# Routing, row sums, key transposes and sink values issued in another order on VectorE, and one more attention tile computed in halves

## The reference

```python
# q, k, v: (4, 8, 768, 64); n_sink = 4; window = 128
scores = scale * np.matmul(q, k.transpose(0, 1, 3, 2))
keep = is_sink | in_window            # in_window: 0 <= rel < window
a = softmax(np.where(keep, scores, -1e9))
x = np.matmul(a, v)                   # as (3072, 512)

a = x @ w1; b = x @ w2                # 512 x 1024 each
x = ((a * b) @ w3) @ w_out            # 1024 x 1024, 1024 x 512

logits = x @ w_gate + modality_bias[modality_id]
e_idx = np.argmax(logits, axis=1)     # one expert of 8 for each token
out[mask] = gate_w[mask, None] * (np.maximum(x[mask] @ w1[e], 0.0) @ w2[e])
```

## Time and profile before

| | us |
|---|---|
| median of three runs | 913.49 |
| lowest and highest run | 912.72, 914.9 |
| the profiled execution's own time | 913.49 |
| its span in the profile | 911.9 |
| TensorE busy | 891.8 |
| VectorE busy | 613.7 |
| ScalarE busy | 383.9 |
| GpSimd busy | 176.9 |

### The profile page before, as it was taken

The page is one execution under the profiler, slowest core; times in us unless marked ns, Lnnn a source line. Parts: engine busy times, 40 slices in busy tenths (PEclk is TensorE's granted clock), DMA queues, the critical chain, the costliest instruction groups (busy, mean ns, idle before and its releaser), DMA issues.

```text
span 911.9 us, 22277 instructions
## 1 busy us (share of the span) xinstructions
PE 891.8 (98%) x8114; PEld 832.1 (91%) x8114; DVE 613.7 (67%) x1469; ACT 383.9 (42%) x933; POOL 176.9 (19%) x289
## 2 busy tenths in 40 slices
PE   7999999999999999999999999999999999999995
PEld 6778999999999999999999999999999999999994
DVE  6776776785776785785786763287666666666655
ACT  3556433342342443333333332251555555444553
POOL 2451112222221241221231221011100000000000
PEclk9999999999999999999999999999999999999998
DMA  7634623123123222222222212234711116111110
GB/s 225 203 116 163 213 66 102 37 92 96 48 87 87 70 71 71 71 83 68 82 71 70 71 48 70 82 140 140 255 46 46 46 58 218 47 47 44 40 40 27
DMA packets 80184, 83.39 MB, mean 91 GB/s; under 512 B 46303, under 2 KB 56543, under 8 KB 80096
## 3 DMA queue, kind: packets, MB, share of 16 engines
q1 hardware_dynamic: 75568, 68.54, 24.4%
q0 software_dynamic: 4240, 13.66, 4.0%
q10 hardware_dynamic: 288, 0.00, 0.0%
HBM read 56.70 MB, written 25.74 MB: 90 GB/s over the span
## 4 chain that ended last, share of the span: by engine, by line
PE 93%; DVE 2%; issue 1%; ACT 1%; DMA 1%; DVEq 0%; ACTq 0%; POOL 0%; SPq 0%; POOLq 0%
PE acc_a L335 7%; PE acc_b L335 6%; PE acc_b L336 6%; PE acc_b L337 6%; PE acc_a L337 6%; PE acc_a L336 6%; PE misc L329 4%; PE misc L331 4%; PE misc L330 4%; PE s_even L949 3%; PE acc_a L329 3%; PE attn L330 2%; PE acc_b L329 2%; PE attn L331 2%; PE attn L329 2%; PE acc_a L331 2%
## 5 line engine op out<-in xcount | busy, mean ns | idle before, releaser
L816 POOL TENSOR_TENSOR probs<-scores,row_inv 128x256 f32<-128x256 f32 x96 | 66.4, 711 | 287.1 <-DVE row_inv L1881 287.1
L1373 ACT ACTIVATE ew<-raw_e 128x1024 fp32r (+1 forms) x100 | 101.3, 1050 | 13.8 <-issue 13.8
L335 PE MATMUL acc_a<-xT_w,w 128*128 128x384 f32 x256 | 90.2, 352 | 0.0
L335 PE MATMUL acc_b<-xT_w,w 128*128 128x384 f32 x256 | 88.0, 344 | 0.4 <-DVE ab L1933 0.4
L336 PE MATMUL acc_a<-xT_w,w 128*128 128x384 f32 x256 | 86.5, 338 | 0.0
L337 PE MATMUL acc_a<-xT_w,w 128*128 128x384 f32 x256 | 86.5, 338 | 0.0
L336 PE MATMUL acc_b<-xT_w,w 128*128 128x384 f32 x256 | 86.5, 338 | 0.0
L337 PE MATMUL acc_b<-xT_w,w 128*128 128x384 f32 x256 | 86.4, 338 | 0.0
L1399 ACT ACTIVATE scores<-scores,neg_max 128x136 f32<-128x136 f32 x192 | 75.8, 398 | 11.3 <-DVE neg_max L1871 11.1
L1373 ACT ACTIVATE uT_w<-ab 128x384 fp32r<-128x384 f32 x64 | 33.4, 521 | 110.5 <-DVE ab L1933 110.5
L2023 DVE TENSOR_TENSOR ew<-raw_e,ew 128x1024 fp32r<-128x1024 f32 x52 | 60.4, 1220 | 28.8 <-ACT ew L1373 28.8
(11 more groups left out here) (371 smaller groups left out, 2966.0 us busy)
## 6 DMA issues: line engine op xcount, KB each, us to landing
raw_e<-in_moe_w SPq DMA_DIRECT2D x24, 512.0 KB, 6.5
raw<-in_moe_w SPq DMA_DIRECT2D x16, 512.0 KB, 6.3
x_in<-routed SPq DMA_DIRECT2D x29, 257.0 KB, 2.9
v_nat<-in_v SPq DMA_DIRECT2D x24, 256.0 KB, 3.0
x_mid<-x_out SPq DMA_DIRECT2D x24, 256.0 KB, 2.0
x_in<-x_mid SPq DMA_DIRECT2D x24, 256.0 KB, 2.7
q_nat<-in_q SPq DMA_DIRECT2D x80, 64.0 KB, 2.2
k_nat<-in_k SPq DMA_DIRECT2D x80, 64.0 KB, 1.9
```

Of the source, the lines that this page charges most:

```text
L335: pe.matmul(o, w_hi, x_hi, start=start, stop=False, skip_group_check=True)
L816: pool.tensor_tensor(probs[:, at, side * HALF:(side + 1) * HALF], scores[:, at, side, SINKS:], row_inv[:, at].unsqueeze(2).broadcast_to([P ...
L1373: return act.activation(o, i, ACT.Copy)
```

## The change

Five things are moved or added. On DVE, `route_place(g - 1)` goes from behind `mlp_uT(g, 0)` to behind `mask_scores(ta, 1)`, and `sums(ta, 0)` goes ahead of `mlp_u(g, 0)`. `take_v_sinks`, which runs in turns 1, 3 and 5, goes from ahead of `mlp_u(g, 3)` to behind `mlp_uT(g, 4)`. `turn_qk` transposes k ahead of q, for 20 tiles; what needs k alone waits for two transposes now, and `scale_q` for all four. Tile 22 is halved, and PE then waits for `first_known` ahead of writing `misc` there.

```diff
--- before.py
+++ after.py
@@ -311,7 +311,7 @@
                 self.par, self.half = i % 2, self.no // 2
                 self.third = self.no // GT
                 self.by_pe = self.no < BY_PE
-                self.halved = self.no >= BY_PE and i >= 1 and self.no != TILES - 2
+                self.halved = self.no >= BY_PE and i >= 1
                 self.second = (s_odd, misc, s_odd)[self.no % GT]
                 self.turns = 4 * (self.no - BY_PE)
                 self.banks_used = self.no + min(self.no, BY_PE)
@@ -801,7 +801,7 @@
                 if t.by_pe:
                     pool.wait_ge(right_empty, 2 * t.no + 1)
                 else:
-                    pool.wait_ge(qk_turned, t.turns + 4)
+                    pool.wait_ge(qk_turned, t.turns + 2)
                 if t.no >= 1:
                     pool.wait_ge(scores_full, 4 * t.no)
                 own = keys[:, t.par, :, 2:5:2, SINKS:]
@@ -932,7 +932,7 @@
                     pe.wait_ge(left_empty, 2 * t.no + 1)
                     pe.wait_ge(right_empty, 2 * t.no + 1)
                 else:
-                    pe.wait_ge(qk_turned, t.turns + 4)
+                    pe.wait_ge(qk_turned, t.turns + 2)
                     pe.wait_ge(left_empty, t.banks_used)
                     pe.wait_ge(right_empty, t.banks_used)
                 pe.wait_ge(k_sink_ready, t.b + 1)
@@ -983,6 +983,8 @@
                     if t.second is misc:
                         pe.wait_ge(wg_taken, FOLD)
                         pe.wait_ge(rank_read, t.third - 1)
+                        if t.third == GROUPS - 1:
+                            pe.wait_ge(first_known, 1)
                     before, own = ((i - 1) % 3, before_probsT), (i % 3, own_probsT)
                     for c in range(PAIRS):
                         for half, (slot, pT), q0, q1 in ((0, own, 0, P), (1, before, 0, P), (0, before, 0, HALF), (1, own, HALF, P)):
@@ -1386,7 +1388,7 @@
                     .then_inc(right_empty, 1)
 
             def scale_q(t):
-                act.wait_ge(qk_turned, t.turns + 2)
+                act.wait_ge(qk_turned, t.turns + 4)
                 act.activation(qT[:, :, :], qT[:, :, :], ACT.Copy, scale=SCALE).then_inc(q_ready, 1)
 
             def exps(t, g):
@@ -1821,18 +1823,18 @@
                 ve.wait_ge(qk_in, 32 * BY_PE + 32 * t.turns + 128)
                 ve.wait_ge(scores_full, 4 * t.no)
                 for a in range(2):
+                    ve.transpose(keys[:, t.par, 2 * a:2 * a + 2, 2:5:2, SINKS:].rearrange("p e m (j f) -> p e f m j", f=4),
+                                 k_nat[:, a * 256:(a + 1) * 256].rearrange("p (f n e) -> p e f n", f=4, e=2)).then_inc(qk_turned, 1)
+                for a in range(2):
                     ve.transpose(qT[:, 2 * a:2 * a + 2, :].rearrange("p e (j f) -> p e f j", f=4),
                                  q_nat[:, a * 256:(a + 1) * 256].rearrange("p (f n e) -> p e f n", f=4, e=2)).then_inc(qk_turned, 1)
-                for a in range(2):
-                    ve.transpose(keys[:, t.par, 2 * a:2 * a + 2, 2:5:2, SINKS:].rearrange("p e m (j f) -> p e f m j", f=4),
-                                 k_nat[:, a * 256:(a + 1) * 256].rearrange("p (f n e) -> p e f n", f=4, e=2)).then_inc(qk_turned, 1)
 
             def take_k_sinks(t, b):
 
                 if t.by_pe:
                     ve.wait_ge(right_empty, 2 * t.no + 1)
                 else:
-                    ve.wait_ge(qk_turned, t.turns + 4)
+                    ve.wait_ge(qk_turned, t.turns + 2)
                 src = keys[:, 0, :, 2:3, SINKS:2 * SINKS].broadcast_to([P, PAIRS, 5, SINKS])
                 ve.tensor_copy(keys[:, 0, :, :, 0:SINKS], src)
                 ve.tensor_copy(keys[:, 1, :, :, 0:SINKS], src).then_inc(k_sink_ready, 1)
@@ -2123,14 +2125,14 @@
                 ta, tb, tc = (group_tile(g + 1, j) for j in range(GT))
                 mask_scores(ta, 0)
                 mask_scores(ta, 1)
+                if g > 0:
+                    route_place(g - 1)
+                sums(ta, 0)
                 mlp_u(g, 0)
                 if g == 0:
                     gate_weights(FOLD - 2)
-                sums(ta, 0)
                 sums(ta, 1)
                 mlp_uT(g, 0)
-                if g > 0:
-                    route_place(g - 1)
                 mlp_u(g, 1)
                 mlp_uT(g, 1)
                 take_probsT(ta, 0)
@@ -2141,8 +2143,6 @@
                 if g == 0:
                     gate_weights(FOLD - 1)
                 sum_x(ta)
-                if tb.i == 1:
-                    take_v_sinks(tb.b)
                 mlp_u(g, 3)
                 mlp_uT(g, 3)
                 mask_scores(tb, 0)
@@ -2151,6 +2151,8 @@
                 mlp_u(g, 4)
                 sums(tb, 1)
                 mlp_uT(g, 4)
+                if tb.i == 1:
+                    take_v_sinks(tb.b)
                 mlp_u(g, 5)
                 mlp_uT(g, 5)
                 take_probsT(tb, 0)
```

## The result

The changed kernel took **923.62 us** (922.93 to 924.85, four runs), beside 913.11 us of the kernel before on the same chip (912.62 to 914.9, four runs). The ratio is 1.0113 with a 95% interval of 1.0095 to 1.0131: 1.1% slower, 10.5 us. The prediction was 922.8 with a range of 918.8 to 926.0, so direction and size came out as forecast. The second was taken 1.5 us too large and the fourth 1.2 us too small, and these two nearly cancel.

A forecast was written before the change was run, and what follows sets the result against it. PE, busy 891.8 of 911.9 us, was taken to bound the kernel. Added waits of 2.5 + 2.4 + 2.5 + 1.95 = 9.35 us on 913.49 gave 922.8 us, range 918.8 to 926.0.

The forecast's parts named there:

- A wait of PE is lost whole.: Throughout PE's program: each wait costs its full length, as read in turn 0, where PE came 0.59 us late.
- Part 1: At `mlp_b(g, 1)`, PE waits for the later `mlp_u(g, 0)`: 0.37 us in six turns, 0.29 in turn 0; 2.5 us together.
- Part 2: Scores of tc tiles 5 to 20: PE waits for q, now transposed last, 0.40 us in each of six; 2.4 us.
- not slower: PE's waits for POOL's sink products, 1.6 us, could close: 4% for a time within 0.2%, 2% for faster.
- let `route_place` take 1.82: DVE ahead of `mlp_u(g, 0)`: `route_place` keeps its length beside POOL, costing 6.8 us there, 927.1 in all; chance 13%.
- let part 1 hide: At `mlp_u(g, 0)`: DVE's short instructions go 0.37 us faster, so PE's wait goes; 918.2 to 920.7 us, chance 10%.
- the assumption of the first paragraph: PE's whole program: no gaps to catch up in, so each wait costs its full length.
- Part 3: `take_v_sinks` beside POOL's `normalise(tb, 1)` in turns 1, 3 and 5: POOL and PE 0.85 us late each, 2.5 us.
- part 3 costs nothing: DVE's gap of 1.04 us takes both instructions of `take_v_sinks`, or both engines get through: 920.3 us, chance 22%.
- Part 4: Values of tile 22: PE waits 2.35 us for `first_known`, halving saves 0.40; 1.95 us net.
- the halved matmuls take 1.50: Values of tile 22, behind the wait for `first_known`: the length of tile 19's halved matmuls, 1.50 us, taken over.

The follow-up runs named there:

- with no wait: The kernel before with tile 22 halved and `first_expert` ahead of `mlp_u(6, 5)`: 912.89 us against 913.05, ratio 0.9998.
- with 1.34: The kernel before with tile 22 halved and `first_expert` between q's and k's transposes of tile 23: 913.99 us against 913.05, ratio 1.0011.
- with 3.88 us: The kernel before with tile 22 halved and `first_expert` behind `mlp_uT(6, 6)`: 919.21 us against 913.05, ratio 1.0068.

## Why the prediction was right, step by step

**"A wait of PE is lost whole."** Nearly, and wrong both ways. Part 1 lost 0.11 more behind each wait of turns 1 to 6, since the second matmul followed the first later; over six turns that is 0.66. Part 2 got 0.73 back at the next wait for POOL. The prediction said that PE has no gaps in which to catch up, and had read the eight waits for POOL a paragraph earlier: those are such gaps. It used them for the rival "not slower" alone.

**Part 1**, predicted 2.5, measured 3.3. Mechanism and terms are confirmed, 1.11 for `route_place` without POOL beside it, 0.29 for the sums, 0.06 to PE, and waits of 0.32 to 0.36 for 0.37. The term was short by the 0.66 above, and by the some 0.4 that turn 2's wait of 0.72 has over the others, from the gap of DVE that stood elsewhere before. The rivals that let `route_place` take 1.82, or let part 1 hide, are both refuted, the one by the 1.11, the other by the waits of 0.32 and more.

**Part 2**, predicted 2.4, measured 0.9. The waits are right (2.24 against 2.4), but 0.73 is given back, and a stretch in PE's scores that the trace of before has by itself doesn't appear with this order. Here the step that failed is the assumption of the first paragraph. The profiled execution of before also had that stretch at 0.94, more than any other trace, and nothing in the prediction looked for it. That the stretch makes up the rest of the 1.5 is a reading of traces and not tested.

**Part 3**, predicted 2.5, measured 2.5, with a half-wrong reason. The model, one engine holding off the other for one instruction at a time, made POOL 0.85 late; it was 0.64. (The long L1847 that it rested on did have a POOL instruction beside it: L797, 2.44 us from 55.81.) It had DVE's loss as the alternative, and both were paid. The size came out because POOL's term was too large by 0.6 over three turns and DVE's was left out, at 0.4 in the trace. So the good size of this part is partly luck. The rival "part 3 costs nothing", at 22%, is refuted.

**Part 4**, predicted 1.95, measured 3.2. The wait was worked out as 2.35 and is 2.32 to 2.33. The saving of 0.40 that was set against it was lost in a larger cost. The step that failed is "the halved matmuls take 1.50": they took 2.77, because TensorE's clock was granted at 0.50 behind the wait. The earlier trace rows have a clock of 1.00 in both windows, and the prediction took tile 19's 1.50 over to a place where PE had just idled, without a word on the clock. The runs with no wait, with 1.34 and with 3.88 us show that it is the wait: 1.00 in the first two, 0.51 behind the last. The term should have been 2.35 - 0.40 + 1.27 = 3.2, and in the changed kernel 0.26 more for the scores behind. The Trainium skill has the rule, in its page "TensorE: Matmul & The Clock Gate", "Part 1: The HAM clock gate": the throttled 1.2 GHz is the state in which an idle TensorE is left, and activity releases it. The clock of 0.50 at the end of the wait of 2.27 us agrees with that, and the 1.00 behind the wait of 1.34 shows that not every idle time leads there. A wait between 1.34 and 2.25 us wasn't tried.

**The sum.** The parts measured one by one are 3.3 + 0.9 + 2.5 + 3.2 = 9.9 us, the whole is 10.5. Each of these has an interval of about 1 us to either side, and some 0.6 of interaction between parts 2 and 3 is in the traces (tiles 8, 14 and 20). So the parts explain the whole within what can be measured. That 922.8 lies 0.8 from 923.62 owes something to chance: part 2's 1.5 too much offsets most of parts 1 and 4's 2.1 too little.

## What to carry to other kernels

When the bounding engine is made to wait, work out what it does behind the wait as well as the wait: a matrix engine that idled for over 2 us came back at half its clock here, one that idled for 1.3 us didn't. Before a wait is booked as lost whole, look for the next wait that the engine already has, since a later arrival shortens it. And an order that starts an answer earlier on a helper engine is worth nothing where nobody waits for that answer, while everything it is moved past is one step later for somebody.

## What the runs showed of the hardware

- The granted clock fell to the lower level in waits of PE of 2.25, 2.27 and 3.88 us, and not in one of 1.34. In this place it made 1.50 us of matmuls take 2.77, 2.78 and 2.74. In the trace the longest wait didn't make it cost more; its repeated times leave this open.
- Two elementwise instructions on DVE and POOL at the same time both got longer: on DVE a cast of 96x512 0.84 for 0.42 and a tensor_tensor of 32x512 0.98 for 0.68, on POOL 1.74 for 1.55 and 1.09 for 0.64. `route_place` took 1.82 beside POOL and 1.11 without it. The copy of `carry_keys` beside the q transposes of DVE did nothing of the kind: 0.60 for 0.61, with 1.14 for the pair of transposes where a pair took 1.13 before. The timeline of the changed kernel at tile 20:

```profile
462.83 1.14 DVE L1829 STREAM_TRANSPOSE qT<-q_nat 128x256 f32<-128x256 f32 x2
...
463.05 0.60 POOL L808 COPY keys<-keys 128x512 f32<-128x512 f32 x1 [4.16 <-DVE keys L1826]
```

- Behind each of part 1's waits, and behind the one wait of the kernel before, the second matmul came 0.28 after the first instead of 0.18.
- DVE idles 0.18 to 0.27 us ahead of its 514th instruction in all 13 traces, with nothing named that it waits for. Where PE waits for what stands there, PE loses some 0.4; elsewhere nothing shows.
- Some stages stretch for a reason that the profile doesn't name: the scores of tiles 8 and 17, by up to 0.94 us, differently from kernel to kernel. Part of this comes back at the next wait: without the stretch in tile 8 PE came 0.20 late at tile 8's sink products. A difference of two traces is therefore read place by place, and a total that differs by less than about 1 us is left to repeated times.
